# Attention and two expert layers on one core: two elementwise products wait for another engine, and the first expert's weights are loaded and split in other places

## The reference

```python
for t in range(S):
    cur = np.einsum('bhd,bhe->bhde', u[None] * kt, vt)
    y[:, :, t] = np.einsum('bhd,bhde->bhe', rt, state + cur)
    state = wt[:, :, :, None] * state + np.einsum('bhd,bhe->bhde', kt, vt)
```

## Time and profile before

| | |
|---|---|
| time, median of 3 runs | 1096.18 us (1095.56 to 1096.74) |
| profiled execution | 1095.09 us, its span 1093.4 us |
| mean granted PE clock | 0.945 of full speed |
| PE busy / weight loads | 968.8 / 860.4 us |
| DVE, ACT, POOL busy | 547.9, 309.5, 354.9 us |
| chain that ended last, over the span | PE 73%, DVE 16%, issue 5%, DMA 3% |

### The profile page before, as it was taken

One profiled execution on the slowest core, in us unless ns is written; L12 is line 12 of the kernel. 1 busy time (PEld: TensorE's weight loads), 2 busy tenths in 40 slices (PEclk: granted clock), 3 DMA queues, 4 the chain that ended last, 5 costly groups with the idle time before them and its releaser, 6 DMA issues.

```text
span 1093.4 us, 24958 instructions
## 1 busy us (share of the span) xinstructions
PE 968.8 (89%) x6314; PEld 860.4 (79%) x6315; DVE 547.9 (50%) x921; ACT 309.5 (28%) x537; POOL 354.9 (32%) x420
## 2 busy tenths in 40 slices
PE   5999898689999999757259999999999999999994
PEld 4888787578889888656148888889888888988884
DVE  8999887765423333224755353443534435353331
ACT  1232223124222222114313242422424233242220
POOL 7333223213322222200524243333423334243222
PEclk9999978899999999968569999999999999999998
DMA  6666752109111111144044225152432524222222
GB/s 226 214 211 212 275 162 91 37 23 331 45 45 43 36 36 43 42 131 168 1 145 146 44 39 162 29 158 43 118 70 42 158 43 145 42 43 43 33 41 36
DMA packets 52965, 108.15 MB, mean 99 GB/s; under 512 B 8304, under 2 KB 34672, under 8 KB 52912
## 3 DMA queue, kind: packets, MB, share of 16 engines
q1 hardware_dynamic: 34624, 71.07, 19.1%
q0 software_dynamic: 14400, 31.55, 14.3%
q10 hardware_dynamic: 3888, 4.89, 1.2%
HBM read 82.67 MB, written 24.82 MB: 98 GB/s over the span
## 4 chain that ended last, share of the span: by engine, by line
PE 73%; DVE 16%; issue 5%; DMA 3%; ACT 1%; POOL 1%; ACTq 0%; SPq 0%; DVEq 0%; POOLq 0%
PE ps L1632 20%; PE ps L1634 19%; PE ps L1633 19%; PE ps L1653 6%; DVE rest L854 3%; DVE grow L869 3%; PE ps L1544 2%; DVE scores L884 2%; DMA w_in<-in_w_T_dram 2%; DVE bonus_v L977 1%; DVE row_mix L1329 1%; PE ps L1558 1%; PE ps L1569 1%; PE ps L1578 1%; PE ps L1506 1%
## 5 line engine op out<-in xcount | busy, mean ns | idle before, releaser
L1341 DVE SCALAR_TENSOR_TENSOR hid_lo<-ps,hid_hi 128x512 fp32r<-128x512 f32 x154 | 106.3, 690 | 297.4 <-ACT hid_hi L794 297.3
L1632 PE MATMUL ps<-weights,hid_hi 128*128 (+1 forms) x616 | 215.2, 349 | 8.2 <-issue 6.7
L1632 PE MATMUL ps<-weights,x_hi 128*128 (+1 forms) x462 | 199.1, 431 | 15.9 <-DVE x_lo L1336 8.4
L1634 PE MATMUL ps<-weights,hid_lo 128*128 (+1 forms) x616 | 208.2, 338 | 0.0
L1633 PE MATMUL ps<-weights,hid_hi 128*128 (+1 forms) x616 | 208.0, 338 | 0.0
L1633 PE MATMUL ps<-weights,x_hi 128*128 (+1 forms) x462 | 184.9, 400 | 0.0
L1634 PE MATMUL ps<-weights,x_lo 128*128 (+1 forms) x462 | 184.4, 399 | 0.0
L789 ACT ACTIVATE h_tok<-ps 128x512 f32<-128x512 f32 x154 | 92.2, 598 | 294.6 <-PE ps L1634 283.8
L794 ACT ACTIVATE hid_hi<-ps 128x512 fp32r<-128x512 f32 x154 | 92.0, 598 | 254.0 <-PE ps L1653 254.0
L646 POOL DMA_INDIRECT out_dram<-sy,dst_now x52 | 92.5, 1778 | 211.0 <-DVE sy L1352 201.9
L1632 PEld LDWEIGHTS ps<-weights,hid_hi 128*128 128x128 f32 x616 | 116.4, 189 | 13.5 <-issue 10.4
(11 more groups left out here) (281 smaller groups left out, 1182.8 us busy)
## 6 DMA issues: line engine op xcount, KB each, us to landing
stage<-in_moe_w_dram SPq DMA_DIRECT2D x20, 1536.0 KB, 9.7
kv_in<-in_kv_T_dram SPq DMA_DIRECT2D x24, 512.0 KB, 5.6
kv_in<-in_kv_T_dram SPq DMA_DIRECT2D x24, 448.0 KB, 3.4
w_in<-in_w_T_dram SPq DMA_DIRECT2D x24, 258.5 KB, 3.8
out_dram<-zeros SPq DMA_DIRECT2D x25, 192.0 KB, 6.7
x_rows<-y_tok ACTq DMA_DIRECT2D x24, 192.0 KB, 4.9
stage<-moe_rows SPq DMA_DIRECT2D x6, 768.0 KB, 4.9
sx<-moe_rows,src_now POOLq DMA_INDIRECT x55, 3.2
```

What stands on the lines that cost most here:

```text
L1341: dve.scalar_tensor_tensor(hid_lo[:, part, :], hT_ps[half], 0.0, hid_hi[:, part, :], ALU.max, ALU.subtract).then_inc(s_hlo[l], 1)
L1632: pe.matmul(out_ps, hi, w_hi, start=first, stop=False)
L1634: return pe.matmul(out_ps, lo, w_hi, start=False, stop=final)
```

## The change

Six edits in one:

1. POOL's `rk` of a chunk also waits for DVE's reciprocal of the chunk after it (`s_inv`), and `k_dec` also waits for `r_dec` of its own chunk (`s_rd`).
2. SP loads the first expert's weights in four parts, w1 in two parts (1 MB and 0.5 MB) and w2 in two halves, one in each of late 2 to 5, each behind that chunk's input loads; before, both were loaded whole in late 3, ahead of that chunk's input loads.
3. ACT makes the high parts in late 6 to 9 instead of 7 to 10, with pieces 0 and 1 in changed order.
4. DVE does `lo` of pieces 2 and 3 in late 10 before and behind `bonus_v`, instead of after the masking.
5. `gate_parts` moves from the last chunk to slot 3, and the picks of chunks 12 to 21 from the last chunk to `first_counts`, where they are done together with the last two.
6. POOL's `first_w2` moves behind the gather of slot 2, and ACT's `row_hot` behind the second slot's hidden values.

```diff
--- before.py
+++ after.py
@@ -216,7 +216,7 @@
 
         HALF = WSZ // 2
         PIECES = [(2, HALF), (2, 0), (1, 0), (1, HALF)]
-        DONE = [[3, 4, 1, 2], [1, 2, 3, 4]]
+        DONE = [[4, 3, 1, 2], [1, 2, 3, 4]]
         w1_raw, w2_raw = stage[:, 0:WSZ], stage[:, WSZ:2 * WSZ]
         sx = [sb(f"sx{i}", [P, CX]) for i in range(2)]
         x_hi, x_lo = sb("x_hi", [P, CC, P], F32R), sb("x_lo", [P, CC, P], F32R)
@@ -408,6 +408,17 @@
                 sp.dma_start(w1_raw.rearrange("p (c f) -> p c f", c=CC),
                              (w1_1, w1_2)[l][e].rearrange("(c p) f -> p c f", p=P)).then_inc(s_w1[l], 16)
 
+            def load_part(q, e):
+
+                if q < 2:
+                    part = slice(0, 2) if q == 0 else slice(2, CC)
+                    sp.dma_start(w1_raw.rearrange("p (c f) -> p c f", c=CC)[:, part, :],
+                                 w1_1[e].rearrange("(c p) f -> p c f", p=P)[:, part, :]).then_inc(s_w1[0], 16)
+                else:
+                    part = slice((q - 2) * FC // 2, (q - 1) * FC // 2)
+                    sp.dma_start(w2_raw.rearrange("p (m n) -> p m n", m=FC)[:, part, :],
+                                 w2_1[e].rearrange("(m p) n -> p m n", p=P)[:, part, :]).then_inc(s_w2[0], 16)
+
             def load_weights(l, e):
                 load_w2(l, e)
                 load_w1(l, e)
@@ -418,11 +429,6 @@
             def attention_loads(b, c, last):
                 g = b * NC + c
                 then = b + (c + NIN) // NC, (c + NIN) % NC
-                if late(b, c) == 3:
-                    sp.wait_ge(s_first, 1)
-                    first = lookup(sp, first_i, 0, E - 1)
-                    load_w1(0, first)
-                    load_w2(0, first)
                 if has_after(b, c, NIN):
                     sp.wait_ge(s_rd, 1 + g + 1)
                     sp.nop(nofuse=True)
@@ -434,6 +440,9 @@
                     sp.wait_ge(s_yT, 1 + g + 1)
                     sp.nop(nofuse=True)
                     load_v(*then)
+                if late(b, c) in (2, 3, 4, 5):
+                    sp.wait_ge(s_first, 1)
+                    load_part(late(b, c) - 2, lookup(sp, first_i, 0, E - 1))
 
             batches(sp, attention_loads)
 
@@ -513,6 +522,8 @@
                 pool.wait_ge(s_krin[i], 16 * fills(b, c))
                 pool.wait_ge(s_rest, g + 1)
                 pool.wait_ge(s_y, 1 + g)
+                if not isinstance(g, int) or g > 1:
+                    pool.wait_ge(s_rd, 1 + g + 1)
                 pool.tensor_tensor(k_dec[c % 2][:, :, :], k_in[i],
                                    rest[c % 2][:, 1:WN + 1].rearrange("p (h t) -> p h t", t=W1)[:, :, 1:W1],
                                    ALU.mult).then_inc(s_kd, 1)
@@ -522,6 +533,8 @@
                 g, i = b * NC + c, c % NIN
                 if not isinstance(g, int) or g > 0:
                     pool.wait_ge(s_bn, g)
+                    if has_after(b, c, 1):
+                        pool.wait_ge(s_inv, g + 2)
                 pool.tensor_tensor(rk[:, :, :], r_in[i], k_in[i], ALU.mult).then_inc(s_rk, 1)
 
             decayed_k(0, 0)
@@ -552,8 +565,6 @@
                         pool.wait_ge(s_xst[u], 16 + 16 * ((EC + 1 - u) // 2))
                     gather_rows(0, 0, 0, early_src, 0)
                     gather_rows(0, 1, 1, early_src, 1)
-                if last:
-                    first_w2()
 
             def first_w2():
 
@@ -658,7 +669,9 @@
                     gather(1, 1, 1)
                 rows_read(1)
                 gather(2, 2, 0)
-                if l == 1:
+                if l == 0:
+                    first_w2()
+                else:
                     pool.wait_ge(s_table[l], 3)
                     split_next(0, split_now)
 
@@ -713,8 +726,8 @@
                 g = b * NC + c
                 if c < NC - 1:
                     carry(b, c + 1)
-                if late(b, c) in (7, 8, 9, 10):
-                    split_piece(0, 0, (2, 3, 0, 1)[late(b, c) - 7])
+                if late(b, c) in (6, 7, 8, 9):
+                    split_piece(0, 0, (2, 3, 1, 0)[late(b, c) - 6])
                 if not last and (c + 1) % NC < NC - 1:
                     k_by_token(*after(b, c))
                 act.wait_ge(s_back, g + 1)
@@ -731,7 +744,7 @@
 
                 which, at = PIECES[q]
                 raw, hi, here = (w1_raw, W1_HI, s_w1[l]) if which == 1 else (w2_raw, W2_HI, s_w2[l])
-                act.wait_ge(here, (n + 1) * 16)
+                act.wait_ge(here, (n + 1) * 16 + (16 if l == 0 and not (isinstance(n, int) and q in (1, 2)) else 0))
                 act.activation(weights[:, bass.ds((n % 2) * 4 * WSZ + hi + at, HALF)], raw[:, at:at + HALF], ACT.Copy)\
                    .then_inc(s_hi[l], 1)
 
@@ -814,6 +827,8 @@
                     def work():
                         if not runs_from(l, s):
                             next_slot(s + 1, lambda q: None)
+                            if s == 0:
+                                row_hot(0)
                             return
                         run = lookup(act, slot_run[l], s, E - 1)
                         later = lookup(act, split_later[l], s, 1)
@@ -829,8 +844,6 @@
                 if l == 1:
                     split_all(0)
                 next_slot(0, lambda q: None)
-                if l == 0:
-                    row_hot(0)
                 slots(act, l, step_slot, peel=PEEL[0] if l == 0 else 0)
 
 
@@ -928,11 +941,11 @@
                     link(dve.tensor_tensor_scan(early_seen[:, :], mine_ps[:, EC:2 * EC], ones[:, 0:EC], 0.0,
                                                 ALU.add, ALU.mult))
                     link(dve.tensor_tensor(early_place[:, :], mine_ps[:, 0:EC], early_seen[:, :], ALU.add))
-                if last:
-                    gate_parts()
-                    pick_best(EC, G - 2)
-                    pick_index(EC, G - 2)
+                if n_late == 10:
+                    split_piece(0, 0, 2, DONE[0])
                 bonus_values(b, c)
+                if n_late == 10:
+                    split_piece(0, 0, 3, DONE[0])
                 dve.wait_ge(s_y, 2 + g + 1)
                 dve.wait_ge(s_bv, 1 + g + 1)
                 dve.tensor_tensor(y_T[:, :, :], y_ps, bonus_v[:, :, :], ALU.add).then_inc(s_yT, 1)
@@ -964,9 +977,6 @@
                        .then_inc(s_earlyread, 1)
                     dve.wait_ge(s_earlyread, 1)
                     early_rows()
-                if n_late == 10:
-                    split_piece(0, 0, 2, DONE[0])
-                    split_piece(0, 0, 3, DONE[0])
 
             def bonus_values(b, c):
 
@@ -1169,8 +1179,8 @@
 
             def first_counts():
 
-                pick_best(G - 2, G)
-                pick_index(G - 2, G)
+                pick_best(EC, G)
+                pick_index(EC, G)
                 dve.sem_inc(s_chosen[0], 1)
 
             def first_places():
@@ -1395,6 +1405,8 @@
                     if s == 2:
                         slot_tables(0)
                         loop_ends(0)
+                    if s == 3:
+                        gate_parts()
                     if s == 3:
                         dve.tensor_tensor(tmp_e[:, :, :], logits[:, :, :], per_expert(best[:, 0, :]), ALU.subtract)\
                            .then_inc(s_ask[0], 1)
```

## The result

The changed kernel takes 1066.59 us in the median of 4 runs (1064.12 to 1067.66); the kernel before takes 1096.33 (4 runs, 1095.56 to 1096.74). The ratio is 0.9726, with a 95% interval of 0.9708 to 0.9745, so 29.7 us less. The forecast was 1066.4 us. The profiled run took 1067.66 us (span 1065.9), which makes it the slowest of its four.

What follows compares the result with a forecast made beforehand. PE was taken to set the pace at 7.07 us per full chunk, with DVE elastic. Gains of 2.6 + 13.9 + 1.05 + 12.3 = 29.8 from 1095.1 give 1065.3, plus 1.1 for the median 1066.4 us; range 1058 to 1077.

Steps and rivals of the forecast that it cites:

- loop: Attention from the start of chunk 1's score products on PE to chunk 13's: 2.6 us less, from PE's idle.
- S(13) to S(22): Late chunks, between the starts of the score products of chunks 13 and 22 on PE: 62.4 for 76.3, 13.9 us less.
- S(22) to M: From the start of chunk 22's score products on PE to the start of the last masking: 1.05 us less.
- M to slot 2: From the start of the last masking to slot 2's first half: 26.2 against 38.5, 12.3 us less.
- the rest: Everything after the start of slot 2: shifted earlier, unchanged in length.
- wait of 1.4 for x_lo before slot 2: Sign in the first slots: PE ready for slot 2 at +24.1 behind the last masking, x_lo only at +25.5.
- Two rivals: Full chunks: DVE sets the pace, 1051 us, chance .04. Late chunks: loads still meet a w, 1074 us, chance .12.
- POOL's two waits: Chunks 2 to 22: moving rk and k_dec off DVE's scans gains only PE's idle, 2.6 us, bounds 0 and 5.7.
- the floor: Late chunks: nine periods of PE's gapless work, 60.5 us, to which .1, .6 and 1.2 are added for 62.4.
- Chunk 22: Start of its score products to the last masking: 13.6 for 14.65 us, 2.0 of PE's idle staying, the clock falling.
- Last chunk and first slots: Behind the last masking: first product at +6.9, picks done at +12.7, slot 1 at +14.6, slot 2 at +26.2; 12.3 us less.
- The clock at short idles: Rival: PE's clock falls at new idles (chunk 18, chunk 22, before slot 2), about 3.3 us each; 1073 us, chance .14.

Runs made afterwards that it cites:

- rowhot_back: The changed kernel with ACT's row_hot back in its old place ahead of the slot loop; 1070.21 us, ratio 0.9774.
- no_waits: The changed kernel without POOL's added waits for rk and k_dec; 1078.03 us, ratio 0.9844.
- w2_back: The changed kernel with POOL's four subtractions (first_w2) back in the last chunk; 1065.41 us, ratio 0.9738.
- w2_splits_back: The changed kernel with first_w2 back in the last chunk and DVE's two splits back behind the last masking; 1071.01 us, ratio 0.9768.
- extra_after: The changed kernel with one more VectorE operation, whose result nothing reads, in each of the 24 chunks; 1076.20 us, ratio 0.9819.
- loads_only: The kernel before with only the four part loads and ACT's high parts one chunk earlier; 1089.41 us, ratio 0.9937.

## Why the prediction was right, and where it wasn't

*The total.* Forecast 29.8 us less on the profiled run, 27.4 measured there, and 29.7 by the medians. That 1066.4 and 1066.59 agree to 0.2 us is luck: the four runs spread by 3.5, and the gains don't all come from the parts that were given them. The steps, forecast and measured: loop 2.6 and 3.3; S(13) to S(22) 13.9 and 12.4; S(22) to M 1.05 and 1.0; M to slot 2 12.3 and 10.15; the rest 0 and 0.5. Shown in the trace as said: the period of 7.07 with idle time on DVE, no wait for w_in (between 110 and 140 us it lands in 5.7 to 7.6 us, against 3.6 to 12.5 before), h_tok of slot 1 free of high_is (rowhot_back gives its price, 2.2 us in the profile), the first product of slot 0 at M + 6.33 (6.9 said), the unchanged rest. Not seen in this profile is the wait of 1.4 for x_lo before slot 2. Two rivals are ruled out: the full chunks did not come under 7, and no scan waited for a load.

*POOL's two waits.* The sizing of the loop holds (3.2 to 3.6 us for 2.6). What failed is the line that DVE's other extras "fit in the 1.1 between 6.0 and 7.07": true with the waits, but I credited the late chunks' gain to the loads, and never asked what those extras cost before. There the waits carry 6.3 to 6.9 of the 12.4 us, the loads 6.4. The sum was right since the floor was worked out with both parts in place; the split over the parts was wrong, and whoever had kept only the loads by my text would have got 6.3 us and not 14. That k_dec's wait matters most in the loop was in the text ("at chunk 1, k_dec no longer stands beside the scan"), that rk's wait alone makes grow longer was not.

*Chunk 22.* 13.6 said, 13.66 measured. The idle before the gate product is 1.77 (2.0 said), and the clock falls behind it, as said. The text put this gain to no part; it is the waits' too, since without them the idle stays 2.77 and the stretch 14.52. The splits in it cost nothing (13.70 without them).

*Last chunk and first slots.* The term that was mis-sized: POOL's four subtractions beside DVE's picks. I priced them as stretching one split from 1.76 to 3, 1.2 us in all. Measured: 3.8 us on logits (4.04 for 0.26), and nothing on the split. The picks and the split end at M + 14.5 and not M + 12.7, PE idles 1.51 before the gathered rows are turned, and works at half clock behind it:
```profile
188.60:194.70 6.10, 5.66 (x16) 4.46 (x17) 5.28 (x17) 0.60 (x1) 1.36 (x3) 0.50 0.13 32
```
So slot 1 starts at +16.7 for 14.6 and slot 2 at +28.36 for 26.2, held by PE and no longer by x_lo. Some 1.1 of the 28.36 is this fall of the clock: in no_waits, with the same operations and the same idle of 1.51, the clock stays at 1.00, slot 2 starts at +27.23, and there PE does wait before it, 1.04 us up to the end of x_lo. With the subtractions away (w2_back) slot 1 starts at +13.98 and slot 2 at +24.88. The edits of this place also hang together: the runs give row_hot 2.2 us of the stretch, the splits none as long as the barrier stands, and picks, gate parts and row_hot 7.4 together with both others undone. The picks and gate parts by themselves were not tried.

*The clock at short idles,* a rival with a chance of .14, came in part: it fell at the 1.14 of chunk 18 and at the 1.51 ahead of slot 1. The first is the whole miss of S(13) to S(22), 63.83 for 62.4: its period was to take 8.3 us with its idle and took 9.96. The window from that idle's end in the changed kernel, and the same window in w2_splits_back, with the same code and the same idle of 1.14, where S(19) to S(20) is 8.44:
```profile
139.16:146.24 7.08, 7.08 (x64) 5.95 (x64) 5.90 (x10) 2.64 (x7) 2.47 (x2) 0.76 0.85 310
...
140.30:147.30 7.00, 7.00 (x83) 6.12 (x84) 6.62 (x12) 3.08 (x7) 2.46 (x2) 1.00 0.89 317
```
So the length of such an idle alone doesn't settle whether the clock falls. The forecast allowed one fall, in chunk 22; the two more cost some 1.7 and 1.1 us, and the loop gave 0.7 more than was forecast.

## What to carry to other kernels

An engine without idle time can be stretched to another one's period, so ask for each kind of stage (full, short, with extras) which engine is late there; one added operation tells it, if the clock is read beside it, and here the answer changed within one loop. Price a part of a change by a run with that part alone and one with all but it: a sum can be right with its parts exchanged. Before a run of GpSimd operations is moved, look at which VectorE operations with two SBUF inputs stand in its new place: a small one can be held for all of it, and whatever is moved ahead of it then brings nothing.

## What the runs showed that I had not expected

- A DVE operation of 0.26 us that reads two SBUF tiles (logits) took 4.04 us beside four POOL subtractions issued back to back (3.90 us): it isn't let in between them. The Trainium skill ("SBUF — State Buffer", Who interferes with whom) says that a DVE instruction with two SBUF inputs contends with a GpSimd instruction that reads SBUF, and that this is an exclusive lock. The trace agrees, with 4.04 for 0.26, and shows that here the wait went over all four subtractions.
- Taking one of two waits away made the other operation's collision worse (grow 1.91 us against 1.62 to 1.73): POOL's two products, 1.27 and 1.19 us, then run without a gap.
- The same idle of PE is followed by a fall of the clock in one profile and not in another. Chunk 18: 1.14 us and a clock of 0.76 over the next 7 us in the changed kernel, 1.14 and 1.00 in w2_splits_back, 1.82 and 1.00 in extra_after. The start of a batch: 0.93 with a fall in loads_only (0.72 between 60 and 66 us), 0.93 without one in the kernel before. What decides it stays open.
- The runs of one kernel differ by 1 to 9 us, along with their mean clock (changed kernel: 1064.12 at 0.959, 1065.91 at 0.957, 1067.26 at 0.953, 1067.66 at 0.952). Single profiles can't be compared to better than that here.
